# Key copies ahead of scatters, zero rows and slabs moved, expert tiles that end at the last token, weights requested in another order

## The chip, the cores and the metric

One core of a Trainium2 chip runs the kernel. The metric is the device time of one execution in microseconds, lower is better; the kernel before has 677.11 us as the median of three runs. A core has five engines with queues of their own: TensorE (PE, matrix products into the eight PSUM banks), VectorE (DVE), ScalarE (ACT), GpSimd (POOL) and SyncE (SP, which here only issues transfers). They meet only at semaphores: `wait_ge(s, n)` holds an engine's queue until s has reached n, and everything behind it in that queue waits too.

## What is computed

Three layers in a row, in float32, for 1536 tokens of 512 features (2 batches of 768, 8 heads of 64):

```python
# 1 attention: 31 neighbours, and maxima of keys / means of values over blocks of 32
k_sum = k.reshape(B, H, nb, 32, D).max(axis=3);  v_sum = v.reshape(B, H, nb, 32, D).mean(axis=3)
scores = concat(where(|i - j| < 16, q @ k.T / 8, -1e9),  q @ k_sum.T / 8 + log(32))
x = softmax(scores) @ concat(v, v_sum)
# 2 mixture of 8 experts, one for each token
e = argmax(normalized(x) @ normalized(emb).T / tau);  gate = softmax(...)[e]
x = gate * (relu(x @ w1[e]) @ w2[e])            # w1: 512 x 1024, w2: 1024 x 512
# 3 a dense layer
h = x @ w_in;  g = (a0 + a1 h + a2 h^2 + a3 h^3) / (1 + |b0||h| + |b1| h^2 + 1e-6);  out = g @ w_out
```

## The kernel before

Matrix products are done in three passes on float32r halves: every operand is split into a high half (a rounding copy) and a low half (the operand less the high half). The weights of one expert, w1 and w2, make a slab of 8192 floats for each partition, and `W[:, slot, HI or LO, :]` holds two slabs. The program is written out by hand for each engine, and the order of its calls is the order of the queue.

**Attention** goes over 12 tiles of 128 queries (T = 0 to 11), each in four pairs of heads; a loop counter `u` counts pairs, and PE runs scores(u), transposes(u-2), products(u-3). For each tile POOL copies windows of keys (`windows(T, half)`, into `KW`, semaphore `kw_done`) and splits queries (`split_q`). SP then copies KW with its partition halves swapped to `KWs` (`swap_windows`, L445 and L446; `kws_in`), and PE's scores wait for it. In its loop over T from 2 on SP issues, in this order: the four swap copies of T, the queries of T+2, four value loads `load_v(T)` (they wait until the products of tile T-2 are done), `load_raw` for an eighth of expert 0's slab, and the next turn begins. Into the same loop POOL has woven `mean_v(2)` (means of the last third of the value blocks), `split_slab0(j)` (the eight pieces of expert 0's slab, each a high copy and a subtraction) and the first scatters. The raw pieces land in two buffers made of rows 7 to 10 of `x_all`, so `make_x` of tiles 7 and 9 waits for splits.

**Routing.** When a tile's row `x_all[:, T, :]` is ready, logits, the chosen expert and a rank give each token a slot in the DRAM tensor `xs`, which has a region of `REGION` = 1664 rows for each expert. `scatter(T)` (L655, an indirect transfer on POOL) writes 128 tokens to their slots. Tiles 0 to 5 are scattered inside the loop, at T = 10 and T = 11:

```python
            SCATTERS = {10: (0, 1, 2), 11: (3, 4, 5)}
            for T in range(3, NT):
                if T > 3:
                    windows(T, 0)
                windows(T, 1)
                ...
                for t in SCATTERS.get(T, ()):
                    scatter(t)
```

An expert's tiles of 128 rows start at its region's first row, so its last tile reads past its last token. The rows there must hold something finite: `clear_tail(e)` (L659) writes 128 zero rows behind the last token of expert e, at `zidx`, after all scatters; four clears go ahead of the loads of tiles 1 and 2 (`load_x`, L692), four behind. Region 0 gets 128 zero rows early (L471), since SP reads its first 128 rows (L502, `x0_in`) before the last two tiles are scattered; PE adds those two tiles by selection matrices (`first_rows`, `stored_rows`, L1695).

**Experts** take MAXT = 19 tiles, in a static loop. For tile i PE runs g1(i+1), the transposes of the hidden values, g2(i); `load_x` fetches rows three tiles ahead. DVE makes the table (`row_of`, `expert_of`, `new_at`, semaphore `tab_ready`) that says which rows and which expert a tile has. If a tile is the first of its expert e, weights are split for expert e+1: ACT makes the high half (`split_hi`, L875), DVE the low half (`split_lo`; its subtraction is L1236, as are those of x and of the hidden values, since all call `lo_of`). A slab comes in four raw chunks of 1 MB, two for w1 (`raw_early`) and two for w2 (`raw_late`), and a buffer is free when its split is done (`half_ready`). SP asks for them (L507):

```python
            load_half(1, 1)
            load_half(2, 0)
            with sp.Fori(2, E - 1) as e:
                load_half(e + 1, 0)
                load_half(e, 1)
```

Half 0 is w1 and half 1 is w2. After its first tile DVE runs `counts()` and `rows_in_order()`, which say where the results of a tile go, between two splits and `x_lo(2)`, the low half of the third tile's x. **The dense layer** follows in 48 units and isn't touched.

Of the kernel before, what the change touches and what calls it, by code (L numbers as in the profile page):

```python
# [38 lines left out]
def moe_mlp_kernel(nc, q, k, v, emb, tau, w1, w2, w_in, w_out, a_coef, b_coef, out):  # L39
# [33 lines left out]
    with ctx:  # L73
# [94 lines left out]
        zidx = ra.take("zidx", [P, E], U32)  # L168
# [7 lines left out]
        iota_p = ra.take("iota_p", [P, E], F32)  # L176
# [10 lines left out]
        raw0 = [x_all[:, NT - 5 + 2 * i:NT - 3 + 2 * i, :].rearrange("p t d -> p (t d)") for i in range(2)]  # L187
# [58 lines left out]
        raw0_in = [sem(f"raw0_in{i}") for i in range(EARLY_SLOTS)]  # L246
# [7 lines left out]
        zero_set, zeroed, zeroed_fourth, zidx_ready = sem("zero_set"), sem("zeroed"), sem("zeroed_fourth"), sem("zidx_ready")  # L254
# [16 lines left out]
        row_ready, sel_ready = sem("row_ready"), sem("sel_ready")  # L271
        scattered, cleared_first, x0_in = sem("scattered"), sem("cleared_first"), sem("x0_in")
# [27 lines left out]
        STACKS, ZERO = UNITS // 2, 6  # L300
# [91 lines left out]
        def _(sp):  # L392
# [54 lines left out]

            def load_raw(j):
                c, half = divmod(j, 2)
                if j >= 2:  # L450
                    sp.wait_ge(w0_ready, j - 1)
                else:
                    sp.wait_ge(ks_mm, 1)
                if c < 2:
                    dst = raw0[half].rearrange("p (k f) -> p k f", f=F)
                    src = w1_v[0, :, c * HALFK + half:c * HALFK + half + 1, :]
                else:
                    at = (c - 2) * HALFF + half * HALFF // 2
                    dst = raw0[half].rearrange("p (k f) -> p k f", f=DM)
                    src = w2_v[0, :, at:at + HALFF // 2, :]  # L460
                sp.dma_start(dst, src).then_inc(raw0_in[half], 16)
# [9 lines left out]
            sp.dma_start(xs[0:P, :], x_all[:, ZERO, :]).then_inc(cleared_first, 16)  # L471
# [13 lines left out]
            for T in range(2, NT):  # L485
# [52 lines left out]
        def _(pool):  # L538
# [66 lines left out]
            def split_slab0(j):  # L605
                if j == 0:
                    pool.wait_ge(kt_mm, KG * FILLS)
                    pool.wait_ge(vm_mm, 2)
                pool.wait_ge(raw0_in[j % 2], 16 * (j // 2 + 1))
                dst = W[:, 0, :, j * CH // 2:(j + 1) * CH // 2]  # L610
                G_.tensor_copy(dst[:, HI, :], raw0[j % 2]).then_inc(hi0_done, 1)
                pool.wait_ge(hi0_done, j + 1)
                G_.tensor_tensor(dst[:, LO, :], raw0[j % 2], dst[:, HI, :].bitcast(F32), ALU.subtract)\
                  .then_inc(w0_ready, 1)

            split_q(0)
            windows(0, 0)
# [16 lines left out]
            link(G_.iota(iota_p[:, :], pattern=[[0, E]], base=0, channel_multiplier=1,  # L634
                         allow_small_or_imprecise_dtypes=True))
# [8 lines left out]
            windows(3, 0)  # L644
            mean_v(2)

            SCATTERS = {10: (0, 1, 2), 11: (3, 4, 5)}
# [10 lines left out]
            def clear_tail(e, done):  # L658
                G_.indirect_dma_start(out=xs, out_offset=bass.IndirectOffsetOnAxis(ap=zidx[:, e:e + 1], axis=0),  # L659
                                      in_=VA[:, 0, :], in_offset=None).then_inc(done, 16)  # L660

            for T in range(3, NT):
                if T > 3:
                    windows(T, 0)
# [3 lines left out]
                if T - 3 < 2 * CHUNKS:  # L668
                    split_slab0(T - 3)
# [1198 lines left out]
```

## Time and profile before

| | |
|---|---|
| median of 3 runs | 677.11 us (674.66 to 678.0) |
| profiled execution | 679.31 us |
| its span, first to last instruction | 677.8 us |
| mean granted clock of TensorE | 0.987 of 2.4 GHz |
| PE busy / DVE / ACT / POOL | 95% / 70% / 60% / 23% |
| chain that ended last: PE / DMA / ACT / POOL | 79% / 6% / 3% / 3% |

How to read it: PE is busy almost always and carries 79% of the chain that ended last, so time is to be had only where PE waits or where its clock is low. The attention takes roughly the first 150 us, the experts up to 400 us and the dense layer the rest. A wait is named by the instruction that ended last before it, and a line can be that of a helper; DMA-issuing instructions don't count as busy. Times in the rows are microseconds from the start of the span.

### The profile page before, as it was taken

Reading aid. Unit: us, or ns where it says so; the run is one execution under the profiler, and the core shown is the slowest. Engines: PE = TensorE matmul, PEld = TensorE weight load, DVE = VectorE, ACT = ScalarE, POOL = GpSimd, SP = SyncE. Lnnn points to the kernel's source line nnn. Section 1 sums busy time; section 2 is a strip of 40 time slices with the busy share of each in tenths; the row PEclk is TensorE's granted clock in tenths of the full one; section 3 lists DMA queues with packets and bytes.
Section 4 is the critical chain, followed back from the end, with each engine's and each line's share of the span. In section 5 each row is a group of like instructions: output and inputs, shape, how many; then the busy total and the mean of one; then the engine's idle time right before and its main releaser. Section 6 shows DMA issues by size and latency. Waiting matters only on the chain.

```text
span 677.8 us, 11272 instructions
## 1 busy us (share of the span) xinstructions
PE 645.6 (95%) x3377; PEld 538.7 (79%) x3377; DVE 473.8 (70%) x944; ACT 405.5 (60%) x762; POOL 155.5 (23%) x198
## 2 busy tenths in 40 slices
PE   5898999788899999999999999999999999999997
PEld 4687999786787788888888888888888888888885
DVE  6875667466766963143234288999898899898886
ACT  6576677536466764343244377776676666766663
POOL 3658878435000122301003002001020000100000
PEclk9999999789899999999999999999999999999999
DMA  8988998559749993284116401001010000000001
GB/s 295 251 195 189 209 228 182 184 186 348 252 147 360 329 370 91 47 285 168 63 47 207 152 16 62 1 16 32 16 62 2 15 1 1 31 33 0 1 1 62
DMA packets 57610, 87.07 MB, mean 128 GB/s; under 512 B 33016, under 2 KB 33032, under 8 KB 56400
## 3 DMA queue, kind: packets, MB, share of 16 engines
q1 hardware_dynamic: 50656, 66.10, 32.9%
q0 software_dynamic: 6448, 20.22, 8.8%
q8 instruction: 31, 0.51, 0.3%
q14 instruction: 27, 0.22, 0.1%
q10 hardware_dynamic: 448, 0.02, 0.0%
HBM read 63.54 MB, written 13.74 MB: 114 GB/s over the span
## 4 chain that ended last, share of the span: by engine, by line
PE 79%; DMA 6%; ACT 3%; POOL 3%; issue 3%; DVE 3%; SPq 1%; another core or an unknown queue 1%; ACTq 0%; POOLq 0%; DVEq 0%
PE bank L1776 20%; PE bank L1791 19%; PE bank L1718 13%; PE bank L1739 13%; PE bank L1490 7%; PE bank L1564 2%; PE bank L1590 2%; DMA raw_late<-in_moe_w_dram 2%; DMA kraw<-in_k_dram 1%; ACT weights L875 1%; PE bank L1592 1%; PE bank L1613 1%; DMA xg<-x_by_slot 1%; DVE weights L1236 1%; DMA qraw<-in_q_dram 1%
## 5 line engine op out<-in xcount | busy, mean ns | idle before, releaser
L1776 PE MATMUL bank<-X2T,weights 128*128 128x512 f32 x576 | 143.1, 397 | 0.0
L1791 PE MATMUL bank<-weights,G 128*128 128x512 f32 x576 | 139.4, 391 | 1.8 <-DVE G L1236 1.8
L1791 PEld LDWEIGHTS bank<-weights,G 128*128 128x128 f32 x576 | 108.0, 188 | 26.4 <-DVE G L1236 2.6
L1776 PEld LDWEIGHTS bank<-X2T,weights 128*128 128x128 f32 x576 | 107.7, 188 | 24.9
L1718 PE MATMUL bank<-weights,XT 128*128 (+1 forms) x432 | 109.9, 404 | 4.3 <-DVE weights L1236 3.7
L1739 PE MATMUL bank<-weights,HT 128*128 (+1 forms) x456 | 111.2, 398 | 0.7 <-DVE HT L1236 0.6
L1739 PEld LDWEIGHTS bank<-weights,HT 128*128 128x128 f32 x456 | 84.2, 188 | 20.1 <-issue 1.1
L1718 PEld LDWEIGHTS bank<-weights,XT 128*128 128x128 f32 x432 | 80.3, 190 | 24.1 <-issue 6.1
L927 ACT ACTIVATE qd<-bank,coef 128x512 f32<-128x512 f32 x48 | 33.0, 688 | 75.9 <-PE bank L1776 75.7
L1236 DVE TENSOR_TENSOR HT<-bank,HT 128x512 fp32r<-128x512 f32 x38 | 24.5, 685 | 67.3 <-ACT HT L955 49.6
L827 ACT ACTIVATE es<-es,nmx 128x184 f32<-128x184 f32 x96 | 42.7, 445 | 31.8 <-DVE nmx L1120 30.2
L1120 DVE CUSTOM_DVE_ANT_0 es<-bank,mask 128x184 f32<-128x184 f32 x96 | 31.5, 342 | 36.5 <-PE bank L1564 32.5
L1236 DVE TENSOR_TENSOR weights<-raw_late,weights 128x2048 f32 (+2 forms) x20 | 41.5, 2078 | 22.2 <-ACT weights L875 22.1
L699 POOL DMA_DIRECT2D y_in_order<-yo x19 | 10.6, 557 | 188.9 <-ACT yo L983 177.6
L1380 DVE SCALAR_TENSOR_TENSOR qd<-sq,absb,qd 128x512 f32<-128x512 f32 x48 | 36.0, 751 | 23.1 <-ACT sq L928 23.1
L1236 DVE TENSOR_TENSOR weights<-raw_early,weights 128x2048 f32 (+2 forms) x20 | 40.7, 2074 | 5.3 <-ACT weights L875 4.6
L875 ACT CAST weights<-raw_late 128x2048 f32 (+1 forms) x16 | 30.5, 1914 | 18.8 <-DMA raw_late<-in_moe_w_dram 18.8
L955 ACT CAST HT<-bank 128x512 fp32r<-128x512 f32 x36 | 19.3, 591 | 35.9 <-PE bank L1490 35.9
L935 ACT ACTIVATE pb<-bank,ncoef 128x512 f32<-128x512 f32 x48 | 37.8, 787 | 0.0
L1397 DVE SCALAR_TENSOR_TENSOR pb<-pb,ncoef,rr 128x512 f32<-128x512 f32 x48 | 36.1, 752 | 1.7
L1390 DVE SCALAR_TENSOR_TENSOR pb<-pb,ncoef,bank 128x512 f32<-128x512 f32 x48 | 35.9, 748 | 1.7
L937 ACT ACTIVATE rr<-qd,onep 128x512 f32<-128x512 f32 x48 | 34.7, 723 | 1.5 <-DVE qd L1380 1.5
(239 smaller groups left out, 1091.1 us busy)
## 6 DMA issues: line engine op xcount, KB each, us to landing
raw_early<-in_moe_w_dram SPq DMA_DIRECT2D x14, 1024.0 KB
raw_late<-in_moe_w_dram SPq DMA_DIRECT2D x14, 1024.0 KB, 9.0
KWs<-KW SPq DMA_DIRECT2D x48, 184.0 KB, 4.5
y_in_order<-yo POOLq DMA_DIRECT2D x19, 256.0 KB
xg<-x_by_slot POOLq DMA_DIRECT2D x18, 256.0 KB, 6.0
x_all<-in_moe_w_dram SPq DMA_DIRECT2D x8, 512.0 KB, 5.3
qraw<-in_q_dram SPq DMA_DIRECT2D x12, 256.0 KB, 6.3
kraw<-in_k_dram SPq DMA_DIRECT2D x2, 1024.0 KB, 9.9
```

The lines of the kernel that those rows point to most:

```text
L827: A_.activation(e_, e_, ACT.Exp, bias=nmx[:, slot:slot + 1], scale=-1.0, accum_out=sums[:, T % 2, 2 * p + i:2 * p + i + 1]).then_inc(exp_d ...
L875: A_.copy(W[:, bass.ds(other, 1), HI, c * CH:(c + 1) * CH].rearrange("p s n -> p (s n)"), raw[c]).then_inc(half_hi[c // PER], 1)
L935: A_.activation(pb[s], h, ACT.Identity, bias=ncoef[:, 2:3], scale=ncoef[:, 3:4]).then_inc(lin_done, 1)
L1236: return V.tensor_tensor(out_, src, hi.bitcast(F32), ALU.subtract)
L1380: V.scalar_tensor_tensor(q_, h2, absb[:, 1:2], q_, ALU.mult, ALU.add).then_inc(q_done, 1)
L1390: V.scalar_tensor_tensor(g_, g_, ncoef[:, 1:2], h, ALU.add, ALU.mult).then_inc(h_read, 1)
L1397: V.scalar_tensor_tensor(g_, g_, ncoef[:, 0:1], r_, ALU.add, ALU.mult).then_inc(g_sb, 1)
L1490: return T_.transpose(dst, src, ident[0:rows, 0:rows])
L1718: last = T_.matmul(bank[half][:, :], x_t(i)[:, xa, kc * P:(kc + 1) * P], weights(par, wa, kc * F + half * BANK), start=(kc == 0 and n_ == ...
L1739: last = T_.matmul(bank[5][:, :], HT[:, ha, fc * P:(fc + 1) * P], weights(par, wa, KC * F + fc * DM), start=(fc == 0 and n_ == 0), stop=(f ...
L1776: last = T_.matmul(bank[6 + f % 2][:, :], W[:, 0, wa, kc * F2 + f * P:kc * F2 + (f + 1) * P], X2T[c % 2][:, xa, kc * C_TOK:(kc + 1) * C_TO ...
L1791: last = T_.matmul(bank[tt][:, :], G[:, f % 2, ga, tt * P:(tt + 1) * P], W[:, 1, wa, f * DM:(f + 1) * DM], start=(f == 0 and n_ == 0), sto ...
```

## The change

1. Zero rows. The early zeroing of region 0 and all `clear_tail`s go. SP writes 128 zero rows at the start of each of the eight regions (`zero_region`) in its turns T = 8, 9 and 10; scatter 0 and `make_x(ZERO)` wait for all eight. The zero row is now `x_all[:, 10, :]`, set by POOL early on.
2. Tiles end at the last token. A tile's first row is the smaller of its old one and (last token - 127), but not below the region's start. This costs five steps more in the table on DVE, `zidx` goes, and `row_of` has a semaphore of its own, `row_at_ready`; POOL loads tiles 1 and 2 on it and on all scatters.
3. POOL's order. windows(3, 1) and split_q(4) go ahead of mean_v(2). Slab piece j is split in tile j+4 (before: j+3), the last one among the scatters. All scatters come after the last key copies.
4. Slab pieces land in the place of their low half (`in_low`), eight places in all, and are split there. SP asks for piece j in turn j+3 (before: two in turn 2, then one in each turn up to 8). `make_x` no longer waits for splits.
5. Weights. SP asks for w2 of e before w1 of e+1, and for the last w2 before w_in.
6. DVE, first tile. split_lo(0,1,1) moves from ahead of the first tile into it, x_lo(2) goes ahead of counts() and rows_in_order().

```diff
-        raw0 = [x_all[:, NT - 5 + 2 * i:NT - 3 + 2 * i, :].rearrange("p t d -> p (t d)") for i in range(2)]
+        in_low = Region(base + SLAB * 4).take("raw_in_low", [P, SLAB], F32)
+        raw0 = [in_low[:, j * CH // 2:(j + 1) * CH // 2] for j in range(2 * CHUNKS)]
...
-        STACKS, ZERO = UNITS // 2, 6
+        STACKS, ZERO = UNITS // 2, NT - 2
+        ZEROED_AT = {8: (0, 1, 2), 9: (3, 4, 5), 10: (6, 7)}
...
+            def zero_region(e):
+                sp.dma_start(xs[e * REGION:e * REGION + P, :], x_all[:, ZERO, :]).then_inc(cleared_first, 16)
+
             def load_raw(j):
                 c, half = divmod(j, 2)
-                if j >= 2:
-                    sp.wait_ge(w0_ready, j - 1)
-                else:
-                    sp.wait_ge(ks_mm, 1)
+                sp.wait_ge(kt_mm, KG * FILLS)
+                if c == CHUNKS - 1:
+                    sp.wait_ge(vmean_ready, KG)
...
-            sp.dma_start(xs[0:P, :], x_all[:, ZERO, :]).then_inc(cleared_first, 16)
...
                 load_v(T)
-                if T == 2:
-                    load_raw(0)
-                    load_raw(1)
-                if 2 <= T - 1 < 2 * CHUNKS:
-                    load_raw(T - 1)
+                if 0 <= T - 3 < 2 * CHUNKS:
+                    load_raw(T - 3)
+                if T in ZEROED_AT:
+                    sp.wait_ge(zero_ready, 1)
+                    for e in ZEROED_AT[T]:
+                        zero_region(e)
...
             with sp.Fori(2, E - 1) as e:
+                load_half(e, 1)
                 load_half(e + 1, 0)
-                load_half(e, 1)
+            load_half(E - 1, 1)
             load_win(0)
-            load_half(E - 1, 1)
...
             def split_slab0(j):
                 if j == 0:
-                    pool.wait_ge(kt_mm, KG * FILLS)
-                    pool.wait_ge(vm_mm, 2)
-                pool.wait_ge(raw0_in[j % 2], 16 * (j // 2 + 1))
+                    pool.wait_ge(kmax_ready, KG)
+                pool.wait_ge(raw0_in[j], 16)
...
             split_q(0)
+            pool.wait_ge(eT_mm, 1)
+            G_.memset(x_all[:, ZERO, :], 0.0).then_inc(zero_ready, 1)
...
             windows(3, 0)
+            windows(3, 1)
+            split_q(4)
             mean_v(2)
...
                 if T == 0:
-                    pool.wait_ge(cleared_first, 16)
+                    pool.wait_ge(cleared_first, 16 * E)
...
-            for T in range(3, NT):
-                if T > 3:
-                    windows(T, 0)
+            for T in range(4, NT):
+                windows(T, 0)
                 windows(T, 1)
                 if T + 1 < NT:
                     split_q(T + 1)
-                if T - 3 < 2 * CHUNKS:
-                    split_slab0(T - 3)
-                for t in SCATTERS.get(T, ()):
-                    scatter(t)
+                    split_slab0(T - 4)
+            for T in range(NT - 6):
+                scatter(T)
+            split_slab0(2 * CHUNKS - 1)
...
             scatter(NT - 1)
-            pool.wait_ge(zero_set, 1)
-            pool.wait_ge(zidx_ready, 1)
-            for e in range(AHEAD):
-                clear_tail(e, zeroed)
-            clear_tail(AHEAD, zeroed_fourth)
-            pool.wait_ge(scattered, 16 * NT)
-            pool.wait_ge(tab_ready, 1)
+            pool.wait_ge(row_at_ready, 1)
...
+                if i == 1:
+                    pool.wait_ge(scattered, 16 * NT)
...
-                if T in (NT - 5, NT - 3):
-                    dve.wait_ge(w0_ready, 2 * CHUNKS - (1 if T == NT - 5 else 0))
...
+            link(V.scalar_tensor_tensor(final, rank[0:1, 0, :], -float(P), thr[0:1, :, 0], ALU.add, ALU.max))
+            link(V.tensor_tensor(rise, final[:, 1:E], final[:, 0:E - 1], ALU.subtract))
...
-            link(V.tensor_scalar(row_of[0:1, :], start, float(P), None, ALU.mult))
+            link(V.tensor_tensor(gone, done, rise.unsqueeze(1).to_broadcast(tab), ALU.mult))
+            link(V.tensor_reduce(limit, gone, AX.X, ALU.add))
+            link(V.tensor_scalar(start, start, float(P), None, ALU.mult))
+            link(V.scalar_tensor_tensor(start, limit, final[:, 0:1], start, ALU.add, ALU.min))
+            V.tensor_copy(row_of[0:1, :], start).then_inc(row_at_ready, 1)
...
+                split_lo(0, 1, 1)
+                x_lo(1)
                 split_lo(0, 1, 2)
-                x_lo(1)
                 split_lo(0, 1, 3)
-                counts()
-                rows_in_order()
                 new1, e1, other1 = after
                 with dve.If(new1):
                     split_lo(e1, other1, 0)
                 x_lo(2)
+                counts()
+                rows_in_order()
```

## Rows read from the trace of the kernel before

**Rows 1.** PE's waits over the span: engine, line, releaser, total us, times, longest
```profile
PE bank L1564 <- DMA KWs<-KW: 4.0, 3, 2.1
```

**Rows 2.** PE's timeline, attention: start, us, engine, line, operation, [idle before <-releaser]
```profile
54.08 0.32 PE L1564 MATMUL bank<-KW,QS 128*128 128x184 f32 x1 [1.13 <-DMA KWs<-KW]
...
64.59 0.32 PE L1564 MATMUL bank<-KW,QS 128*128 128x184 f32 x1 [2.08 <-DMA KWs<-KW]
...
108.02 0.32 PE L1564 MATMUL bank<-KW,QS 128*128 128x184 f32 x1
...
148.52 2.05 PE L1695 MATMUL bank<-ident,xg 128*128 128x128 f32 x8
```

**Rows 3.** POOL's timeline, 45 to 152 us
```profile
46.20 5.46 POOL L581 TENSOR_TENSOR vraw<-vraw 128x1024 f32<-128x1024 f32 x5
...
54.79 1.04 POOL L611 CAST weights<-x_all 128x1024 fp32r<-128x1024 f32 x1
...
58.22 1.38 POOL L601 CAST KW<-KTc 128x640 fp32r<-128x640 f32 x2
...
147.67 0.96 POOL L655 DMA_INDIRECT x_by_slot<-x_all,slot_id  x1 [4.80 <-DMA xg<-x_by_slot]
...
150.60 0.96 POOL L659 DMA_INDIRECT x_by_slot<-VA,zidx  x1 [0.30 <-issue]
```

**Rows 4.** Three stretches: length, busy (count) by engine, clock, DMA share, GB/s
```profile
60.00:80.00 20.00, 17.92 (x149) 17.63 (x148) 11.59 (x61) 12.61 (x44) 17.65 (x20) 0.91 0.96 221
98.00:106.00 8.00, 7.82 (x71) 7.55 (x70) 5.29 (x28) 5.58 (x20) 5.45 (x7) 1.00 1.16 219
130.00:140.00 10.00, 9.07 (x64) 8.67 (x64) 5.32 (x29) 6.13 (x22) 0.96 (x1) 0.78 0.08 30
```

**Rows 5.** The chain that ended last, 100 to 240 us: start, us, what
```profile
124.93 3.96 another core or an unknown queue
...
153.13 4.15 DMA x_by_slot<-VA,zidx
...
158.92 6.97 DMA xg<-x_by_slot
```

**Rows 6.** PE's timeline, hand-over and experts
```profile
165.94 0.66 PE L1490 MATMUL bank<-ident,xg 128*128 128x128 f32 x4 [1.60 <-DMA xg<-x_by_slot]
...
177.32 4.35 PE L1718 MATMUL bank<-weights,XT 128*128 x12 [1.89 <-DVE weights L1236]
...
205.27 3.06 PE L1718 MATMUL bank<-weights,XT 128*128 x12 [1.04 <-DVE weights L1236]
...
231.53 3.05 PE L1718 MATMUL bank<-weights,XT 128*128 x12 [0.81 <-DVE weights L1236]
```

**Rows 7.** SP's timeline: its transfers as issued
```profile
97.56 0.85 SPq L420 DMA_DIRECT2D VA<-in_v_dram  x2
...
101.62 0.60 SPq L446 DMA_DIRECT2D KWs<-KW  x1
...
144.11 0.35 SPq L502 DMA_DIRECT2D xg<-x_by_slot  x1
...
157.40 23.62 SPq L507 DMA_DIRECT2D raw_early<-in_moe_w_dram  x4
181.31 1.00 SPq L507 DMA_DIRECT2D raw_late<-in_moe_w_dram  x2
```

**Rows 8.** DVE's timeline, 140 to 215 us
```profile
151.91 0.29 DVE L1262 TENSOR_REDUCE r<-big 1x20 f32<-1x140 f32 x1
...
169.67 2.29 DVE L1236 TENSOR_TENSOR weights<-raw_late,weights 128x2048 fp32r<-128x2048 f32 x1 [1.73 <-ACT weights L875]
...
176.43 0.68 DVE L1236 TENSOR_TENSOR XT<-bank,XT 128x512 fp32r<-128x512 f32 x1
```

**Rows 9.** ACT's timeline, 140 to 275 us
```profile
175.53 0.58 ACT L880 CAST XT<-bank 128x512 fp32r<-128x512 f32 x1
```

**Rows 10.** DMA issues of the page: count, KB each, median us to landing
```profile
KWs<-KW SPq DMA_DIRECT2D x48, 184.0 KB, 4.5
```

More of the change, by code:

```diff
@@ L245, in moe_mlp_kernel @@
         raw_in = [sem(f"raw_in{i}") for i in range(CHUNKS)]
-        raw0_in = [sem(f"raw0_in{i}") for i in range(EARLY_SLOTS)]
+        raw0_in = [sem(f"raw0_in{j}") for j in range(2 * CHUNKS)]
         hi0_done, w0_ready = sem("hi0_done"), sem("w0_ready")
@@ L271, in moe_mlp_kernel @@
         row_ready, sel_ready = sem("row_ready"), sem("sel_ready")
+        row_at_ready, zero_ready = sem("row_at_ready"), sem("zero_ready")
         scattered, cleared_first, x0_in = sem("scattered"), sem("cleared_first"), sem("x0_in")
@@ L458, in load_raw @@
                     at = (c - 2) * HALFF + half * HALFF // 2
[L459 removed]
+                    dst = raw0[j].rearrange("p (k f) -> p k f", f=DM)
                     src = w2_v[0, :, at:at + HALFF // 2, :]
[L461 removed]
+                sp.dma_start(dst, src).then_inc(raw0_in[j], 16)
             load_k(0)
@@ L720, in _ @@
             for i in range(1, AHEAD):
-                pool.wait_ge(zeroed, 16 * AHEAD)
                 load_x(i)
-            for e in range(AHEAD + 1, E):
-                clear_tail(e, zeroed)
             for i in range(MAXT):
-                if i == 1:
-                    pool.wait_ge(zeroed, 16 * (E - 1))
-                if i == 0:
-                    pool.wait_ge(zeroed_fourth, 16)
                 if i + AHEAD < MAXT - 1:
@@ L1036, in _ @@
             V.memset(eps_row[:, :], 1e-9)
-            V.memset(x_all[:, ZERO, :], 0.0)
             V.memset(VA[:, :, :], 0.0).then_inc(cleared, 1)
@@ L1243, in _ @@
             counted = bank[7][:, (H + 1) * E:(H + 2) * E]
-            V.tensor_tensor(zidx[:, :], counted, iota_p[:, :], ALU.add).then_inc(zidx_ready, 1)
             link(V.tensor_copy(rank[:, 0, :], counted))
@@ L1252, in _ @@
             link(V.tensor_reduce(ends, cum, AX.X, ALU.add))
+            final, rise = rank[0:1, 1, :], pick[0:1, 0, 0:E - 1]
+            link(V.scalar_tensor_tensor(final, rank[0:1, 0, :], -float(P), thr[0:1, :, 0], ALU.add, ALU.max))
+            link(V.tensor_tensor(rise, final[:, 1:E], final[:, 0:E - 1], ALU.subtract))
             done = big[0:1, :].rearrange("p (i e) -> p i e", e=E)[:, :, 0:E - 1]
             gone = big2[0:1, :].rearrange("p (i e) -> p i e", e=E)[:, :, 0:E - 1]
-            expert, change, start = r12[0:1, 7, :], r12[0:1, 5, :], r12[0:1, 6, :]
+            expert, change, start, limit = r12[0:1, 7, :], r12[0:1, 5, :], r12[0:1, 6, :], r12[0:1, 4, :]
             tab = [1, MAXT + 1, E - 1]
@@ L1331, in rows_in_order @@
                 link(V.tensor_reduce(change, gone, AX.X, ALU.add))
-                link(V.scalar_tensor_tensor(start, expert, -float(REGION // P), start, ALU.mult, ALU.add))
-                link(V.scalar_tensor_tensor(change, start, float(P), change, ALU.mult, ALU.add))
+                link(V.scalar_tensor_tensor(start, expert, -float(REGION), start, ALU.mult, ALU.add))
+                link(V.tensor_tensor(change, start, change, ALU.add))
                 V.tensor_copy(crow_of[0:1, :], change).then_inc(crow_ready, 1)
@@ L1464, in _ @@
             split_lo(0, 1, 0)
-            split_lo(0, 1, 1)
             dve.wait_ge(tab_ready, 1)
```

20 lines of the change are left out of this document (4 added, 16 removed).

## The prediction

> **What bounds the kernel now.** The waits of PE show how small the prize is: over the whole span it stands still 4.0 us for key windows, in three waits [rows 1], and little more for anything else that this change touches. From about 206 us on PE hardly stops, so the change can act on three stretches: the attention loop (32 to 150 us), the hand-over to the experts (150 to 180 us), and the experts with one tile each (180 to 260 us).
>
> In PE's timeline of the attention loop two waits carry the releaser KWs: 1.13 us ahead of 54.08 and 2.08 us ahead of 64.59 [rows 2]. POOL's timeline says why. Between the two halves of query tile 3 stand the value means (five instructions, 5.46 us) and the split of slab 0 (54.79 to 58.22, 3.43 us) stands ahead of the copies of tile 4, which start at 58.22 [rows 3]. After the second wait the granted clock is 0.91 over 20 us [rows 4]: about 3.6 us of it ran at the lower of the two levels (1.2 GHz against 2.4), and 0.09 x 20 = 1.8 us are lost, though no instruction got longer by its work.
>
> From 124.93 the chain books 3.96 us as "another core or an unknown queue" [rows 5]; PE, ACT and DVE all stood still in it. I can't name the cause. Behind it, too, the clock is low: 0.78 over ten us, 2.2 us lost [rows 4].
>
> In the hand-over PE waits 1.60 us for the second tile's rows at 165.94 and 1.89 us at 177.32; the twelve matmuls that follow take 4.35 us where 3.06 is usual (205.27) [rows 6]. The label of the second wait, "weights L1236", is a helper's line; what ends just before it is the low half of x, 176.43 + 0.68 = 177.11 [rows 8]. In the experts' part the waits are 1.04 us at 205.27 and 0.81 us at 231.53 [rows 6].
>
> **The change, part by part.** *Means and slabs behind the key copies.* windows(3,1) follows windows(3,0) at once, some 6 us sooner. The two early slab loads (1 MB) leave SP's queue ahead of the copies of tile 3, so the 1.13 us go. For tile 4 the slab of 3.43 us leaves POOL's path: the copies start at about 54.8, not 58.22; SP swaps 1.2 us later, a swap lands 4.5 us after issue [rows 10], so about 60.9 against a PE that would be there at 62.5 - 1.1 = 61.4. The 2.08 us go too, and with them the 1.8 us of clock: together -5.0 us. Bounds: 0, if another input is as late, to -5.0. I take -5.0, because from tile 5 on POOL waits for the queries of each tile and so has slack of its own.
>
> *Zero rows by SP.* Eight writes of 256 KB move into the turns of tiles 8, 9 and 10, three, three and two. One issue costs SP 0.60 us [rows 7], so a turn of three puts 1.8 us and 786 KB ahead of the swap of the next tile. Turns 9 and 10 also get a slab load of 512 KB which they didn't have. How near is that? In turn 8 the value loads start at 97.56, the second swap copy is issued at 101.62 [rows 7], lands 4.5 us later at 106.1, and PE uses it at 108.02 [rows 2]: slack 1.9 us. The 1.8 us of issue eat it. The DMA engines are full there (share 1.16 at 219 GB/s, 98 to 106 us) [rows 4], and 786 KB at that rate take 3.6 us. So the cost for turn 8 is between 0 (the swap isn't held up by writes that go to another memory) and about 3.5 us; turns 9 and 10 start from the same delay and add only their excess. All three together: 0 to +5.0. I take +2.0, under half, because 219 GB/s is a rate of 256-byte packets and the zero rows are packets of 2 KB.
>
> By the Trainium skill, "DMA: Bandwidth & Descriptors", section on queues, rings and completion order, each DMA engine consumes the descriptors of one ring in ring order; by that the swap stands behind every zero row of its turn and the cost would be the upper bound, 3.5 us or more in turn 8. The trace of before has no zero write ahead of a swap, so it can't say; this is the first rival below.
>
> *Scatters behind the last key copies.* windows(11) now starts about 3 x 1.26 = 3.8 us sooner (an indirect write is 0.96 + 0.30 [rows 3], and three stood ahead of those copies). PE wasn't seen waiting on those copies, so I book nothing for them directly. Whether the unnamed pause goes with the crowd of scatters, swaps and value loads at 120 to 127 us is open: bounds 0 and -(3.96 + 2.2) = -6.2 us. But the tail of POOL limits it. Scatter 0 now waits for all eight zero writes. A turn is 8.3 us (64.59 to 108.02 less the 1.8 of clock, over five), so turn 10 begins at 97.56 + 16.6 - 5.0 + 1.5 = 110.7; value loads and slab take 3.5 (97.56 to 101.1), two zeros 1.2, landing 4.5: 119.9. Then six scatters 7.6, slab 7 3.4, four scatters 5.0: 135.9, and the last of them lands 4.15 after its issue [rows 5], at 138.8. SP's read of the first rows took from 144.11 [rows 7] to 147.67 [rows 3], so it would end at 142.4. PE wants these rows at 148.52 - 5.0 + 2.0 = 145.5 with the pause, 139.4 without [rows 2]. So only about half of the 6.2 us can be kept. Value: half a chance of 3.1, -1.4 us, rounded down.
>
> *Tiles end at the last token, no clears of tails.* Four clears (1.26 us each, first at 150.60 [rows 3]) and the wait for the landing of the third, 4.15 us from 153.13, stood ahead of the load that was issued at 158.92 and took 6.97 us [rows 5]. Now the load waits for row_at_ready and scatter 11. The table on DVE has at most ten small steps of 0.29 + 0.04 us behind 152.20 (end of L1262 [rows 8]) and x_lo of 0.7: 156.2 at the latest, register load 1.5, landing 6.97: 164.7. PE wants it at 165.94 - 1.60 = 164.34. So -1.6, bounds -1.2 and -1.6; without 2 MB of clears beside it the load should be quicker. tab_ready comes at most 1.7 us later; relu(0) and tile_at wait for it, covered by the first tile's matmuls.
>
> *x low half ahead of counts.* XT's high half ends at 175.53 + 0.58 = 176.11 on ACT and the low half began at 176.43 [rows 8, 9]: -0.3 us. The rest of the 1.89 us (relu, copy, subtraction) stays, so I leave the low clock behind it where it is: 0, bound -1.3 (4.35 - 3.06). split_lo(0,1,1) moves behind the HT halves, to about 162 to 164.3, and g1(1) wants it only at 169: covered; its raw chunk comes free 4.7 us later, and its successor is needed at 176.
>
> *Weights in the order of use.* SP stood from 157.40 for 23.62 us on the next expert's w1 before it could ask for this expert's w2 at 181.31 [rows 7], though that buffer was free from 169.67 + 2.29 = 172 [rows 8]. Now w2 is asked for ten us sooner. The late w2 held ACT and DVE in tile 2 and later, and so the w1 split that PE waits for: 1.04 + 0.81 = -1.9 us. Bounds 0 to -1.9. The w1 chunks move behind two w2 requests of 0.4 us each in the same queue, free sooner than needed. In-place splitting and the memset on POOL cost nothing: the shapes are the same, and the memset lies where POOL waits for the first key maxima.
>
> **Sum** against the profiled execution, 679.31 us (span 677.8 and 1.5 around it): -5.0 + 2.0 - 1.4 - 1.6 - 0.3 - 1.9 = -8.2, so 671.1. That execution lies 2.20 above the median of the runs, 677.11; carried over, 668.9. If the pause is what the profile has more, the term of -1.4 isn't to be had from the runs: 677.11 - 6.8 = 670.3. I forecast 669.6.
>
> **The rivals.**
> 1. *The zero writes hold the swaps up.* For it: full DMA engines, slack of 1.9 us only. Against: 2 KB packets, and copies that land in 4.5 us in that same traffic. The attention gain is mostly eaten: term +5.0 and no -1.4, and a wait like that ahead of 64.59 brings a slow clock of up to 1.8: 669.6 + 3.0 + 1.4 = 674.0, up to 675.8.
> 2. *The pause goes as a whole or the clock stays up,* zeros cheap: 669.6 - 2.0 - 1.7 - 1.3 = 664.6. For it: its place is where the change thins the traffic. Against: POOL's tail.
> 3. *The weights' order changes nothing:* in the experts' stretch one stage of DVE and ACT bounds, and only its label moves. 669.6 + 1.9 = 671.5.
> 4. *Slower:* DMA bandwidth becomes the bound in turns 8 to 10. 2.10 MB of zeros and 1.05 MB of slabs at 219 GB/s are 14.4 us. In place of +2.0 that gives 669.6 + 12.4 = 682.0. It decides from 10.2 us of cost on; against it: before, too, 4 MB of slabs passed in this loop without a wait of PE.
>
> **How the numbers follow.** Forecast 0.48 (its own range 667 to 672.5), rival 1 0.22, rival 2 0.14, rival 3 0.11, rival 4 0.05. A measurement of this kernel can tell about 0.5% (3.4 us) from no change, so faster means under 673.7: forecast, rivals 2 and 3, and 0.09 of rival 1, 0.82; within it the rest of rival 1, 0.13; slower 0.05. The range leaves out rival 4 and the ends of rivals 1 and 2: 663.5 to 675.
>
> **What would show it.** No KWs wait over 0.5 us before 70 us and the clock at 1.00 there; PE's waits of turns 9 to 11 give the zeros' price; xg released without a wait; raw_late requested near 170 us and no wait for the split at the two places in the experts' part. Wrong it would be made by KWs waits over 3 us at tile 9 or 10, by a PE that stands before the stored rows of tile 0 for more than 4 us, or by a pause that comes elsewhere.

## The result, and the profile after

The changed kernel is slower: 692.68 us in the median of four runs (691.81 to 694.28), against 675.98 us for the kernel before, run beside it. The ratio is 1.0251, with a 95% interval of 1.0213 to 1.0289. The forecast was 669.6 us, and neither its range nor the slower rival reaches the result. The profiled execution took 691.81 us with a span of 690.1, so 12.3 us more than the span of before.

First PE's waits over the whole span, after (engine, line, releaser, total us, times, longest):

```profile
PE bank L1704 <- DVE XT L1216: 19.2, 2, 9.8
...
PE bank L1550 <- DMA KWs<-KW: 2.9, 4, 1.1
PE bank L1681 <- DMA xg<-x_by_slot: 2.2, 1, 2.2
```

Two waits make 19.2 us, under a name that before had none of size. The second and third line are small and stand where the prediction looked. PE's timeline of after puts all of them in place:

```profile
94.49 0.32 PE L1550 MATMUL bank<-KW,QS 128*128 128x184 f32 x1 [0.79 <-DMA KWs<-KW]
...
103.40 0.32 PE L1550 MATMUL bank<-KW,QS 128*128 128x184 f32 x1 [0.47 <-DMA KWs<-KW]
...
112.91 0.32 PE L1550 MATMUL bank<-KW,QS 128*128 128x184 f32 x1 [1.06 <-DMA KWs<-KW]
...
141.90 2.08 PE L1681 MATMUL bank<-ident,xg 128*128 128x128 f32 x8 [2.23 <-DMA xg<-x_by_slot]
...
158.72 0.66 PE L1476 MATMUL bank<-ident,xg 128*128 128x128 f32 x4 [0.36 <-DMA xg<-x_by_slot]
...
169.81 3.06 PE L1704 MATMUL bank<-weights,XT 128*128 x12 [1.60 <-issue]
...
194.95 2.96 PE L1704 MATMUL bank<-weights,XT 128*128 x12
...
229.69 4.58 PE L1704 MATMUL bank<-weights,XT 128*128 x12 [9.40 <-DVE XT L1216]
...
253.83 4.47 PE L1704 MATMUL bank<-weights,XT 128*128 x12 [9.84 <-DVE XT L1216]
...
267.84 2.97 PE L1704 MATMUL bank<-weights,XT 128*128 x12
```

and of before, where it is needed beside [rows 6]:

```profile
244.13 2.97 PE L1718 MATMUL bank<-weights,XT 128*128 x12
...
256.65 2.97 PE L1718 MATMUL bank<-weights,XT 128*128 x12
```

Read it against [rows 2, 6] by the same piece of work. Query tiles and expert tiles are both counted from 0. The key windows of tile 9 start at 103.40, before at 108.02: 4.6 us ahead. The stored rows of tile 0 at 141.90 against 148.52: 6.6 ahead. The rows of expert tile 1 at 158.72 against 165.94: 7.2. The first product of expert tile 4 at 194.95 against 205.27: 10.3 us ahead. Up to there the kernel did what the forecast said, and more. The first product of expert tile 6 is at 229.69 against 231.53, and of 10.3 us 1.8 are left; tile 7 (253.83 against 244.13) loses them too. Two waits of 9.40 and 9.84, the twelve matmuls behind each that take 4.58 and 4.47 in place of 3.06, less the 0.81 us that before had at tile 6, turn 10.3 us ahead into 11.2 behind at tile 8 (267.84 against 256.65), which stays and is 12.3 at the end of the span.

Busy time in two windows of 20 us of after (length, busy and count by engine, clock, DMA share, GB/s):

```profile
220.00:240.00 20.00, 10.60 (x46) 8.46 (x45) 10.97 (x7) 10.41 (x10) 1.08 (x2) 0.74 0.47 177
240.00:260.00 20.00, 10.16 (x43) 7.93 (x42) 10.23 (x6) 10.51 (x11) 2.61 (x3) 0.74 0.46 159
```

PE, DVE and ACT are each busy for about half of the time, and the DMA engines for under half: none of them is full. ACT's timeline names what is waited for, SP's says when it was asked for, DVE's when its buffer came free. ACT:

```profile
222.00 1.90 ACT L858 CAST weights<-raw_early 128x2048 f32 x1 [9.82 <-DMA raw_early<-in_moe_w_dram]
...
246.17 1.90 ACT L858 CAST weights<-raw_early 128x2048 f32 x1 [10.29 <-DMA raw_early<-in_moe_w_dram]
```

SP:

```profile
209.67 2.57 SPq L509 DMA_DIRECT2D raw_late<-in_moe_w_dram  x2
212.54 1.00 SPq L509 DMA_DIRECT2D raw_early<-in_moe_w_dram  x2
```

DVE:

```profile
202.21 4.50 DVE L1216 TENSOR_TENSOR weights<-raw_early,weights 128x2048 f32 x2 [0.38 <-DVE gate_id L1299]
206.62 0.69 DVE L1216 TENSOR_TENSOR XT<-bank,XT 128x512 fp32r<-128x512 f32 x1
207.23 4.49 DVE L1216 TENSOR_TENSOR weights<-raw_late,weights 128x2048 f32 x2
...
224.09 2.29 DVE L1216 TENSOR_TENSOR weights<-raw_early,weights 128x2048 f32 x1 [9.16 <-ACT weights L858]
226.59 2.29 DVE L1216 TENSOR_TENSOR weights<-raw_early,weights 128x2048 f32 x1 [0.21 <-ACT weights L858]
228.80 0.68 DVE L1216 TENSOR_TENSOR XT<-bank,XT 128x512 fp32r<-128x512 f32 x1
```

The buffer of w1 (raw_early) was free chunk by chunk at 204.5 and 206.7 (the middle and the end of 202.21 + 4.50), when DVE had split what lay in it. SP asked for the next w1 only at 212.54, because it stood in the same program behind the next w2, whose buffer (raw_late) DVE frees from 209.5 on. A request that could have left at 204.5 left 8 us later and landed at 222.0.

PE's wait carries the name of the low half of x (XT), and the last lines say why: in DVE's program that piece (228.80 to 229.48) stands behind the split of w1, as the high half does in ACT's, and PE starts at 229.69. So late w1 holds up the next tile's x whether or not that tile needs the new w1. At 253.83 it doesn't: DVE splits w1 in a tile's turn if the next tile begins an expert, and behind the split of 248.25 to 253.02 there is none until 299.45, so tile 7 has the same expert as tile 6.

### The profile page after: what moved, and what is told of

It is laid out like the page before. It is cut to its first block, busy times and chain, and to the rows that moved or that the text cites. A ratio compares the mean times of both kernels' runs of the same rounds, so it can differ in the third digit from the quotient of the medians.

```text
span 690.1 us, 11274 instructions
## 1 busy us (share of the span) xinstructions
PE 645.7 (94%) x3377; PEld 538.2 (78%) x3377; DVE 473.8 (69%) x948; ACT 405.0 (59%) x762; POOL 148.0 (21%) x189
## 4 chain that ended last, share of the span: by engine, by line
PE 76%; DMA 9%; DVE 3%; ACT 3%; issue 3%; SPq 3%; POOL 2%; DVEq 0%; ACTq 0%; POOLq 0%
PE bank L1762 20%; PE bank L1777 19%; PE bank L1704 13%; PE bank L1725 13%; PE bank L1476 7%; DMA raw_early<-in_moe_w_dram 3%; PE bank L1550 2%; DMA xg<-x_by_slot 2%; DMA KWs<-KW 1%; DMA x_by_slot<-x_all,slot_id 1%; DMA kraw<-in_k_dram 1%; PE bank L1576 1%; ACT weights L858 1%; POOL x_by_slot L657 1%; DVE weights L1216 1%
## 5 line engine op out<-in xcount | busy, mean ns | idle before, releaser
L1704 PE MATMUL bank<-weights,XT 128*128 (+1 forms) x432 | 111.8, 409 | 20.8 <-DVE XT L1216 19.2
L1704 PEld LDWEIGHTS bank<-weights,XT 128*128 128x128 f32 x432 | 81.9, 194 | 41.3 <-issue 22.4
L858 ACT CAST weights<-raw_early 128x2048 f32 (+1 forms) x16 | 30.1, 1912 | 22.6 <-DMA raw_early<-in_moe_w_dram 22.6
L966 ACT COPY yo<-bank 128x512 f32<-128x512 f32 x18 | 10.6, 590 | 44.1 <-PE bank L1725 44.1
```

The costliest lines, as they stand in the source:

```text
L858: A_.copy(W[:, bass.ds(other, 1), HI, c * CH:(c + 1) * CH].rearrange("p s n -> p (s n)"), raw[c]).then_inc(half_hi[c // PER], 1)
L1704: last = T_.matmul(bank[half][:, :], x_t(i)[:, xa, kc * P:(kc + 1) * P], weights(par, wa, kc * F + half * BANK), start=(kc == 0 and n_ == ...
```

## The experiments

Ratios are to the kernel before, run beside each set on the same chip; its medians there were 681.34 (e1 to e4), 682.28 (e5 to e8), 681.94 (e9 to e11) and 674.87 us (e12, e13). Times of different sets are therefore compared by their ratios. The times expected for e1 to e3 were reckoned from 675.98 us; as ratios, 672 is 0.994, 696 is 1.030 and 671 to 672 is 0.993 to 0.994.

### e1: the changed kernel with the old order of weights

```
             with sp.Fori(2, E - 1) as e:
-                load_half(e, 1)
                 load_half(e + 1, 0)
-            load_half(E - 1, 1)
+                load_half(e, 1)
             load_win(0)
+            load_half(E - 1, 1)
             load_win(1)
```

> The changed kernel, its weight requests back in the old order (w1 of e+1 ahead of w2 of e). Theory (the new order makes the request for w1 of e+1 stand in SP's queue until a w2 buffer is free, and PE pays for it): PE's waits of 9.40 and 9.84 us at 229.69 and 253.83 go, with the 3.0 us of low clock behind them, and 1.9 us of waits for late w2 return: 692.7 - 22.3 + 1.9 = 672, raw_early requested within 1 us of the end of its split. Rival (POOL's new order or the in-place slabs make the splits slow): the two waits stay and the time is over 685.

678.59 us, ratio 0.9961 (0.993 to 0.9992). Both long waits are gone: in the experts' part PE's longest is 1.95. The whole loss of 2.5% is undone by these lines, and the other parts together are worth 0.4%.

### e2: the kernel before with the new order alone

The same edit, the other way round, on the kernel before.

> The kernel before with the new order of weight requests alone. Theory: two or more waits of PE of 9 to 10 us each for the third and fourth expert with one tile, 676 + 22.3 - 1.9 = 696. Rival (the new order does harm only together with the earlier hand-over): 674 to 678.

701.65 us, ratio 1.0285 (1.0215 to 1.0355). PE's waits of this kernel:

```profile
PE bank L1718 <- DVE XT L1236: 20.3, 3, 9.7
```

The line that in after had 19.2 us stands here with 20.3, without any other part of the change; 9.24 and 9.71 of it are at tiles 6 and 7 (239.85 and 264.01). e1 and e2 together show that the order of the requests is the cause: take it out and the loss goes, put it in alone and it comes.

### e3: w2 of expert 2 first, then the old order

w2 of expert 2 and w1 of expert 3 change places, and from expert 3 on the old order stands. Against e1:

```
+            load_half(2, 1)
+            load_half(3, 0)
-            with sp.Fori(2, E - 1) as e:
+            with sp.Fori(3, E - 1) as e:
```

> The changed kernel; only w2 of expert 2 is requested ahead of w1 of expert 3, all later ones in the old order. Theory: the buffer of w2 is free early only there, since experts 0 and 1 have three tiles; so 671 to 672, up to 1 us faster than all in the old order, and no wait over 1.5 us in the experts' part. Rival (any w2 ahead of a w1 costs a landing time of 9 us): 680 or more.

673.92 us, ratio 0.99 (0.9851 to 0.9949). SP's timeline of this kernel, where the new order helps and then where the old one does:

```profile
165.90 2.57 SPq L509 DMA_DIRECT2D raw_late<-in_moe_w_dram  x2
170.31 27.25 SPq L509 DMA_DIRECT2D raw_early<-in_moe_w_dram  x4
197.84 1.00 SPq L509 DMA_DIRECT2D raw_late<-in_moe_w_dram  x2
207.66 2.55 SPq L509 DMA_DIRECT2D raw_early<-in_moe_w_dram  x2
212.65 2.57 SPq L509 DMA_DIRECT2D raw_late<-in_moe_w_dram  x2
```

The w2 that before left at 181.31 [rows 7] leaves at 165.90. The w1 that in after left at 212.54 leaves at 207.66, ahead of w2, and is there in time: behind 180 us PE waits only 0.47 and 0.61 us in the experts' part. The interval ends at 0.9949, so the gain over the kernel before is clear of noise, but it is under 2%. Only e9 (0.9897) has as low a ratio, and the intervals don't tell the two apart.

### e4: the zero rows in turns 3 to 6

```
-        ZEROED_AT = {8: (0, 1, 2), 9: (3, 4, 5), 10: (6, 7)}
+        ZEROED_AT = {3: (0, 1), 4: (2, 3), 5: (4, 5), 6: (6, 7)}
```

On top of e3.

> As the one before, and the eight zero rows in turns 3 to 6, two in each, instead of turns 8 to 10. Theory (the late zero writes cost KWs waits of 1.5 us at tiles 9 and 10, and hold scatter 0 for 6.75 us, from which PE's 2.23 us ahead of the stored rows come, with low clock behind): PE's wait at the stored rows goes, 3 to 5 us faster than the one before, 667 to 669. Rival (the traffic is only moved, and the earlier turns pay): the KWs waits come at tiles 4 to 7, no difference over 1 us.

679.48 us, ratio 0.9952 (0.9914 to 0.9991). The 3 to 5 us that I expected are not there. The first scatter no longer waits for zero rows, in e3 6.76 us, but starts only 1.1 us sooner (119.09 against 120.22): POOL ends its last key copies at 118.91 and in e3 at 113.46, since from 55 us on its waits for queries and slab pieces add up to 15.6 us, in e3 to 10.4. PE's key waits are 4.3 us in seven places, in e3 2.9 in four, so the writes cost no less in the early turns. In the profile PE also waits 3.64 us at 128.62 for ACT, which stood still, and the runs spread from 672.8 to 682.2 us; what part of the 0.5% against e3 belongs to the zero rows is not shown.

### e5: means and slabs back ahead of the key copies

On top of e3: the means return to their place between the halves of windows(3), and the slabs are split one turn sooner, with `load_raw(T - 2)` and `split_slab0(T - 3)`.

> This is the kernel of e3_one_pair_ahead (673.92 us) with one more part of the change taken back: the third k-mean product and the slab splits stand between the query and key copies again, one turn earlier, and no slab is left for after the scatters. My theory: the swaps of turns 3 and 4 are asked for later, the key waits before 80 us come back (the first tile of the kernel before waited 1.1 and 2.1 us at 54.08 and 64.59 us) and with them the granted clock of 0.91 between 60 and 80 us; the prediction put this part at 5.0 us, so 677 to 680 us. Rival A: the time is only passed on to the stretch behind 120 us, where the fixed order of scatters and reads decides, and the kernel stays within 2 us of 673.9. Rival B: it is faster by 1 to 2 us, since the last slab no longer stands between the scatters of tiles 5 and 6 (671.5 to 673).

684.79 us, ratio 1.0051 (1.0015 to 1.0087). Against e3's 0.99 that is 1.5%, about 10 us, where I had priced the part at 5.0. PE's timeline, as far as it differs:

```profile
64.53 0.49 PE L1550 MATMUL bank<-KW,QS 128*128 128x184 f32 x1 [3.70 <-DMA KWs<-KW]
...
120.20 0.32 PE L1550 MATMUL bank<-KW,QS 128*128 128x184 f32 x1 [2.38 <-DMA KWs<-KW]
```

The wait is back at the place of [rows 2] and is larger, 3.70 for 2.08; the clock between 60 and 80 us is 0.83. A second one of 2.38 comes at tile 11, and DVE's longest stop is 6.63 us (table below), for 2.32 in e3. All key waits together are 6.9 us for 2.9 in e3, and 0.83 over 20 us loses 3.4 us, so an estimate of 7.4 of the 10 us is accounted for. The rest lies where the stops are, and whether the order of POOL's work brings it isn't shown.

### e6: the kernel before with e3's order alone

> The kernel before with only the weights' order of e3_one_pair_ahead: w2 of expert 2 and w1 of expert 3 change places, all later experts keep the old order. My theory: the weight waits of tiles 1 to 3 of the kernel before (1.04 us at 205.27, 0.81 us at 231.53) shrink below 0.6 us each and no wait of 9 us appears, so 1 to 2 us less than the kernel before run beside it: ratio 0.997 to 0.9985. Rival: the order gives nothing even here, ratio within 0.9985 to 1.002. That it would come out over 1.01, as the whole new order did (1.0285), both exclude.

678.63 us, ratio 0.9932 (0.99 to 0.9965): 4.6 us, more than twice what I had expected of it. From e1 to e3 the same edit gave 0.9961 to 0.99, so the medians repeat it. The profiles do so only in part. From the first expert product to the end of the span e1 takes 524.1 us and e3 and e11 520.3 and 520.9, so 3.2 to 3.8 us are gained where the order acts. The kernel before takes 524.4 and 525.3 (e8), but e6's profile 524.2, with a wait of 0.97 us at 230.96 that I had expected below 0.6. That execution, 681.31 us, is the slowest of e6's ten; where its median gains 4.6 us is open.

### e7 and e12: all scatters behind the attention

```
                 if T == 0:
                     pool.wait_ge(cleared_first, 16 * E)
+                    pool.wait_ge(pv_mm, PAIRS * NT)
```

On top of e3. In e12 the last slab of expert 0 is also split ahead of the scatters, as in e10.

> The kernel of e3_one_pair_ahead, but the first scatter waits until the last tile's score-times-value products are through, so that no scatter is under way during the last two tiles' attention. It asks where the pause of 3 to 4 us comes from in which all three engines stand still between 119 and 134 us of five of the profiles so far. Theory S, the scatters in flight cause it: no pause of over 2 us between 115 and 140 us, and the granted clock of 130 to 140 us is above 0.7. Rival V, the value and weight loads of the last turns cause it, or something outside this core's queues: a pause of 3 to 4 us can show here too. Twelve scatters of some 0.9 us each and their landing then stand on the path to the first expert tile, so both give a slower kernel by 6 to 14 us: 680 to 688 us.

> The kernel of e3_one_pair_ahead with all scatters behind the last tile's products, as in e7_scatters_last, but with the last slab of expert 0 split ahead of them, so that TensorE does not wait 12 us for that slab. If scatters in flight are what stops VectorE and ScalarE (2.3 to 6.6 us in all profiles but e7 and the changed kernel's own): again no idle stretch of over 2 us put down to a remote or unseen releaser before 136 us, granted clock 1.00 from 120 to 130 us. The time then says what the scatters cost behind attention: twelve at 1.27 us end at 151 us instead of 145, so the first tile's rows come at 150 to 153 us and the kernel takes 675 to 680 us. If the stops come anyway, e7 was luck and the cause lies outside the scatters.

e7 took 684.68 us in one run and e12 681.52 us, ratio 1.0092 (1.006 to 1.0124). In neither did DVE or ACT stop during attention without a shown releaser. e7 lost time besides because PE stood 12.05 us at 147.30 for the last slab, which e12 splits earlier. Windows of e7, then of e3, between 120 and 140 us:

```profile
120.00:130.00 10.00, 10.00 (x91) 9.63 (x89) 8.06 (x45) 7.35 (x28) 0.00 (x0) 1.00 0.38 80
```

```profile
120.00:130.00 10.00, 8.17 (x68) 7.58 (x66) 4.64 (x25) 5.13 (x18) 8.17 (x8) 0.95 0.59 192
130.00:140.00 10.00, 9.15 (x44) 8.59 (x43) 3.78 (x20) 3.94 (x13) 5.34 (x6) 0.50 0.33 120
```

With no scatter PE is busy for all ten microseconds; in e3 it runs 68 matmuls where it ran 91, and the clock falls to 0.50, the lower level of the two, behind it. But the changed kernel, with scatters in the same window, runs 81 at clock 1.00. What e7 and e12 save is lost again at the rows: PE's timeline of e12

```profile
144.74 2.08 PE L1677 MATMUL bank<-Sel,x_all 128*128 128x128 f32 x8 [5.96 <-DVE Sel L1162]
...
153.67 2.08 PE L1684 MATMUL bank<-ident,xg 128*128 128x128 f32 x8 [6.77 <-DMA xg<-x_by_slot]
```

### e8 and e13: the kernel before and the changed kernel again

> The kernel before, unchanged, profiled once more, to see whether the pause of 3.9 us at 129 us and the start of the expert tiles (153.4 us in the first profile) come again in the same place. If they are properties of the schedule: the pause within 1 us of 129.5 and the first expert matmul within 1 us of 153.4. If they differ from one execution to the next: a pause elsewhere between 118 and 135 us or none, and a first expert matmul between 148 and 157 us, with the time following it (675 to 685 us).

> The changed kernel, unchanged, once more beside e12 on the same chip. Its one profile is the only one with scatters in the last turns and no stop of VectorE or ScalarE of over 2 us without a shown releaser. If that belongs to its schedule, the second profile has none either (first expert matmul near 147.8 us, 691 to 694 us). If it was one execution's luck, a stop of 2 to 6 us can appear between 119 and 138 us and the time can reach 698 us. The two waits of 9.4 and 9.8 us at 229.69 and 253.83 us stand in both cases.

e8 took 681.11 us. Its pause is 3.17 us long and ends at 132.24, and the first expert product starts at 154.28, against 153.39 in the first profile. Its key waits have other sizes and places: 0.46 us at 53.45, 1.51 at 63.40 and a new one of 1.56 at 81.66, six in all with 5.7 us, and the clock between 60 and 80 us is 1.00. At the place of the 1.89 us of [rows 6] stands:

```profile
178.13 3.07 PE L1718 MATMUL bank<-weights,XT 128*128 x12 [1.61 <-issue]
```

So a kernel's own waits of one to two microseconds, and the slow clock behind them, differ from one execution to the next.

e13 took 693.18 us, ratio 1.026 (1.0193 to 1.0327), with the long waits at 232.11 (9.52) and 256.28 (8.91), and again no stop in the attention.

### e9, e10 and e11: when the scatters may start, and e3 again

```
                 if T == 0:
                     pool.wait_ge(cleared_first, 16 * E)
+                    pool.wait_ge(v_in[(NT - 1) % 2], 64 * (NT // 2))
```

e9 is e4 with this wait. e10 is e3 with it, and with `split_slab0(2 * CHUNKS - 1)` moved ahead of the first scatter. e11 is e3 unchanged.

> The kernel of e4_zeros_early (679.48 us, profile with a pause of 3.64 us at 128.62 and the granted clock at 0.50 behind it), with one wait more on GpSimd: the first scatter waits until the last tile's value loads have landed. In the profiles so far the engines stood still for 2.3 to 6.6 us where the last value loads were requested 2.4 to 11 us behind the first scatter, and did not with the scatters behind the loads or all of them last (e7). Theory: the pause needs value loads behind scatters; here no pause of over 1.5 us of TensorE, VectorE or ScalarE between 115 and 140 us, granted clock over 0.85 there, first expert matmul at or before 150 us, 671 to 675 us. Rival: the pause comes whenever scatters run during the last two turns of attention, and stays at 3 to 4 us: 677 to 682 us.

> The kernel of e3_one_pair_ahead (673.92 us) with the last slab of expert 0 split ahead of the scatters and the first scatter waiting for the last value loads. Theory: the stops of 2.3 us at 126 and 129 us of that profile and its granted clock of 0.50 between 130 and 140 us go; the scatters of tiles 0 to 9 end near 138 us as before, since the 3.4 us of the slab leave their middle; first expert matmul at 146 to 149 us, 669 to 672.5 us. Rival: scatters that start 4 us later push the rows of the first tile out and the kernel stays at 673 to 677 us.

> The kernel of e3_one_pair_ahead once more, beside the other two on the same chip, to see how far its first time (673.92 us, four runs) and its profile repeat. If the stretch from 118 to 145 us varies from one execution to the next as it did between the two profiles of the kernel before, 672 to 680 us with a pause of 0 to 4 us; if the order of requests fixes it, 673 to 675.5 us and again two short stops instead of one long one.

e9: 675.61 us, ratio 0.9897 (0.985 to 0.9945). e10: 678.06, ratio 0.9944 (0.9908 to 0.9981). e11: 673.13, ratio 0.9904 (0.9864 to 0.9944), so e3 repeats. The theory on the value loads falls with both: e9 has a stop of 2.90 us, and in e10 they were requested at 119.39 and had landed before the first scatter at 124.56, and the longest stop but one of the study came. e10's time lies above what its theory and its rival allowed. e11 has one stop of 4.08 us where e3 had two of 2.3, so this stretch differs between executions of one kernel. DVE's timeline, then ACT's, of e10:

```profile
137.57 0.56 DVE L1113 COPY PT<-bank 128x384 f32<-128x384 f32 x1 [6.42 <-remote]
```

```profile
137.71 0.58 ACT L826 COPY xT<-bank 128x512 f32<-128x512 f32 x1 [5.79 <-remote]
```

"Remote" means that the trace has no instruction of this core that released them.

## Why the prediction was wrong

**The step that failed** is "The w1 chunks move behind two w2 requests of 0.4 us each in the same queue, free sooner than needed." I priced the requests by their issue and not by what they wait for. A w2 request waits until the w2 of the expert before has been split, and SP's program is in order, so each w1 waited for that too. Term 6 was bounded at 0 and -1.9 us; in the changed kernel its gain was there up to tile 5, and at tiles 6 and 7 it cost 9.40 + 9.84 us of waits and (4.58 - 3.06) + (4.47 - 3.06) = 2.9 us of clock, 22.2 us together. e1 and e2 show this from both sides; and from the first expert product to the end of the span the two kernels with the whole new order take 18.5 to 21 us more than the kernel before (table below). The evidence lay in [rows 7, 8]: I looked up when the w2 buffer was free for the one pair where it frees early (172 us, nine before its request) and took that for the rule. PE runs the first product of tile t+1 before the second of tile t, and with one tile for each expert ACT and DVE split the next w1 ahead of this w2 (202.21 and 207.23 in DVE's timeline above). So the old order was the order of use, and w1's buffer also comes free first.

**Rival 2** came true in its part on the pause, by luck as far as the runs show: e3 and e11 have the same attention and the pause. **Rival 3** (the order changes nothing) had the right object and no mechanism; rival 4 had the right sign, and its mechanism did not occur: PE's key waits behind the zero rows stayed at 1.06 us or less (at most 1.62, in e1).

**Term 1**, -5.0 us: no key wait between 32 and 70 us, clock 1.00 between 60 and 80 us. At tile 9 PE is 4.6 us ahead though it has lost 0.79 + 0.47 since, so 5.9 us. The mechanism is right: with the old order of POOL's work all four profiles of before, e8, e2 and e6 wait for keys at tile 4 (2.08, 1.51, 1.92 and 4.02 us), and the changed kernel, e13, e1, e3 and e11 don't. The size holds for the profile that I read; 1.8 us of it were the clock, which in e8 and e2 stayed at 1.00 there. (The swap of tile 4 would by its own terms land at 54.8 + 1.2 + 4.5 = 60.5, not 60.9; nothing hangs on it.) e5, which takes this part back, costs more.

**Term 2**, +2.0 us: 0.79 + 0.47 + 1.06 = 2.3 us at tiles 8 to 10. The first of these stands ahead of the first zero row (SP issues it at 95.86), so 1.5 us come behind zero rows. In e13, e3, e11 and e1 the waits at tiles 9 and 10 add up to 2.0, 2.0, 2.1 and 2.7 us. Right in size. By the Trainium skill, "DMA: Bandwidth & Descriptors", section on queues, rings and completion order, the descriptors of one ring are consumed in ring order, so the swaps would stand behind the zero rows. The measured waits of 0.47 and 1.06 us are far from the 3.5 us that I had put beside that rule from the rate of small packets. Whether it is the rate that doesn't fit these rows, or the swaps don't wait for all of them, no run here tells.

**Term 3**, -1.4 us: undersized for this profile. The pause was absent in both profiles of the changed kernel. POOL's tail did limit it as worked out: PE reached the stored rows at 139.67 (139.4 was the estimate) and they came at 141.90 (142.4). From tile 9 to there it gained 2.0 us, though 1.06 of key wait fell in between.

**Term 4**, -1.6 us: the wait for the rows of tile 1 fell from 1.60 to 0.36 us, so 1.24, the lower bound. The path was another than the one worked out: POOL stood 5.75 us until 150.64 for the last scatters to land and then issued the load, and the table on DVE wasn't what came last. **Term 5**, -0.3 us: 1.60 in place of 1.89, and the twelve matmuls behind it took 3.06 for 4.35. But the kernel before had the same 1.61 and 3.07 in e8, so this measures nothing of the part.

**The sum without term 6's failure.** With e3's order the kernel has all six parts and the ratio 0.99; the forecast was 669.6 / 677.11 = 0.989. That agreement is partly luck: the edit of e3 was worth 4.1 to 4.6 us by the medians (e1 to e3, e6), not 1.9, and the other five parts 0.4% (e1), not 6.3 us or 0.9%. In the profiles the first expert product comes at 147.2 to 156.7 us with the five parts (changed, e13, e1, e3, e11; mean 150.5) and at 153.4 to 155.6 without (before, e8, e2, e6; mean 154.5), so 4.0 us sooner, and the single gains differ by as much as the stops do.

**What stays open** is the stop. The table gives for each profile the first scatter, the longest idle time of DVE or ACT between 119 and 138 us whose releaser is remote or not shown ("issue"), the start of the first expert product, and the time from there to the end of the span, in which the kernels that share the changed kernel's other parts differ only in the order of the weights; none means that every idle time of over 2 us there is released by an instruction that the trace shows.

| profile | first scatter | stop | first product | from there to the end |
|---|---|---|---|---|
| before | 116.35 | 3.99 | 153.39 | 524.4 |
| e8, before again | 118.06 | 4.62 | 154.28 | 525.3 |
| e2 | 115.25 | 3.81 | 154.73 | 545.5 |
| e6 | 119.03 | 4.38 | 155.57 | 524.2 |
| e1 | 123.26 | 5.93 | 156.65 | 524.1 |
| e4 | 119.09 | 4.81 | 156.69 | 521.3 |
| e3 | 120.22 | 2.32 and 2.31 | 150.94 | 520.3 |
| e11, e3 again | 119.60 | 4.08 | 149.03 | 520.9 |
| e5 | 124.73 | 6.63 | 164.60 | 521.8 |
| e9 | 126.16 | 2.90 | 154.90 | 522.8 |
| e10 | 124.56 | 6.42 | 154.65 | 520.8 |
| changed | 120.56 | none | 147.19 | 542.9 |
| e13, changed again | 122.28 | none | 148.90 | 543.2 |
| e7 | 136.22 | none | 162.25 | 520.6 |
| e12 | 136.37 | none | 158.96 | 520.4 |

Every profile with a stop had scatters under way; with the scatters last there was none, twice. But scatters aren't enough: the changed kernel has them and no stop, twice, and it differs from e3 and e11 only in SP's program for the time behind 160 us. Eleven of thirteen profiles with scatters in the attention have a stop, so two without can be chance, and so can the two with the scatters last. The loads of instruction blocks that the traces show in this stretch (16 KB each) don't sort the profiles either: one starts at 123.01 in e3 and 123.08 in e10, with stops, and at 123.79 in the changed kernel and 124.46 in e7, without. The cause stays open.

## What to carry to other kernels

A request costs its issue and also the wait in front of it, and everything behind it in an in-order program pays that wait: before two requests are exchanged, write down for each when its buffer comes free and when its data are used, for every kind of turn of the loop and not only for the turn in which the profile shows the loss. "Order of use" is read from the timelines, here from the order in which ACT and DVE empty the buffers: a pipelined loop may use the next tile's first operand before this tile's second, and what stands behind a late operand in an engine's program is late too, under its own name. Where one kernel's profiles differ by several microseconds in one stretch, profile the kernel before twice, ahead of pricing a wait in it, and compare stretches that the variation doesn't touch.

## What the runs showed of the hardware

The granted clock fell behind each long wait: the twelve matmuls behind the waits of 9.40 and 9.84 us took 4.58 and 4.47 us, those behind 9.52 and 8.91 in e13 5.48 and 5.42, against 3.06 at the full clock. After the stops in the attention whole stretches of ten microseconds ran at 0.50 (130 to 140 us in e3 and e4, 140 to 150 in e9 and e10), and e4, with a stop of 4.81 us, reached its first expert product 9.5 us later than the changed kernel, which had none (156.69 against 147.19); how much of that is the stop's alone isn't shown. I had expected neither the size of these stops nor that all eleven profiles that have one have scatters under way.
